# Logits of the last chunk from its hidden values and (w_out w_gate), with part of its rows made later

## The chip, the cores and the metric

The kernel runs on one core of one Trainium2 chip. The metric is the device time of one execution in microseconds (us), less is better. TensorE (PE) multiplies, VectorE (DVE) and ScalarE (ACT) work element by element, GpSimd (POOL) does too and issues indirect transfers, SyncE (SP) issues the plain ones. Line numbers (L1206) are those of the kernel before.

## The reference

```python
x = attention(q, k, v, proj)                 # (1536, 512)
h = np.maximum(x @ w_in, 0.0)                # (1536, 2048)
x = h * h @ w_out                            # (1536, 512): the rows y
logits = x @ w_gate                          # (1536, 8)
# Greedy routing by descending logit: each token goes to one expert,
# at most 192 tokens to an expert, ties in index order.
out[mask] = np.maximum(x[mask] @ w1[e], 0.0) @ w2[e]
```

## The kernel before, in words

All of it is one program in three stages: attention, the first layer (h and y), and the eight experts with the routing. The change lies in the first layer and at its join with the experts.

**First layer.** The 1536 tokens are done in four chunks of 384 (`HALF`). A chunk goes over 16 tiles f of 128 hidden columns; g = 16 c + f counts them through. For each tile TensorE does `hidden` (twelve matmuls of 384 columns, L925: two-part products of a weight split in high and low parts) into bank PB[g % 2], and `rows` (nine matmuls of 512 columns, L1206: three token tiles times three part products) which add up in PB[2] to PB[4] over all 16 tiles. The order on TensorE is hidden(g+1), then rows(g). Between the two stand, for each tile:

- ScalarE (`tile`, L929): relu out of the bank (L931) and its square, rounded to the high part h_hi (L933); then the high part of the w_in columns of tile g+2 (L942) and of the w_out rows of tile g+1 (L945). `split_parts` holds these parts, two buffers each.
- VectorE (`hidden`, L1120): the exact square h from the relu (L1122), and h_lo = h - h_hi (L1125), which `rows` waits for (semaphore hls). Both inputs of both instructions are in SBUF.
- GpSimd (`both_low`, L993): the low part of the w_in columns (L949) and of the w_out rows (L953), each one tensor_tensor of 128x512.

In the first tiles of the next chunk ScalarE copies the finished rows out (L1079), TensorE turns them (`turn`, L1220), VectorE copies the columns (L1130), TensorE makes their logits with w_gate (`logits`, L1228), VectorE copies those into L (L1134), and SP stores the rows in HBM (`y_rows`, L986). After the last chunk the same is done with nothing beside it: copies L1114 and L1116, twelve transposes L1281, twelve fp32 matmuls L1289, and the store L989. VectorE also fills the routing's tables, between the fourth and the fifth tile of the last chunk (L1169 to L1180); GpSimd its masks at the end (L1036 to L1049).

**Experts.** A new block starts, at which the engines join. VectorE chooses each token's best expert (L1516 to L1528). The first route goes in 13 steps (`STEPS`): for five digit levels TensorE counts with twelve small matmuls (L1698) what VectorE compared (L1540), VectorE answers (L1548), one more small matmul (L1700); then the places (L1666) and the token list (L1673). TensorE waits for VectorE in most steps; after steps 10 and 11 `keep_warm(5)` has five matmuls that nothing reads (L1778). GpSimd gathers the tokens' rows from `y_rows` (L1406) once all rows are stored and the list is there; SP loads the expert's weights into the places of w_in and w_out. Then TensorE runs expert after expert (L1755, L1769), with the later routes laid into it.

## Time and profile before

| | before |
| --- | --- |
| median of 3 runs | 800.35 us (800.28 to 800.99) |
| the profiled execution | 801.0 us |
| its span in the trace | 799.2 us |
| TensorE, VectorE, ScalarE, GpSimd busy | 97%, 46%, 47%, 50% |
| mean granted TensorE clock | 0.979 of full |

The span is the time from the first to the last instruction of the profiled execution; 1.8 us of the execution's own time lie around it. A line of a timeline has the start, the duration, the engine, the kernel line, what is written and read, and in brackets how long the engine had been idle and what ended that. "x2" is a merged pair. The attention takes the first third, the first layer runs from about 265 to 547 us, the experts from 552 us on.

### The profile page before, as it was taken

The page shows a single profiled execution, that of the slowest core. Times are in us where ns is not written, and L with a number is a line of the kernel's source. Part 1 is how long each engine was busy: PE and PEld are TensorE (multiplying, and loading weights), DVE is VectorE, ACT ScalarE, POOL GpSimd, SP SyncE. Part 2 cuts the span into 40 slices and gives each one's busy share as a digit, 9 for nine tenths or more (in the row PEclk, how much of TensorE's full clock was granted, in tenths as well). Part 3 has the DMA queues.
Part 4 walks back from the last instruction along what each step waited for, and adds up shares of the span by engine and source line. Part 5 has one row for each costly group of instructions (what it writes and reads, how often), then busy time and mean ns, then how long its engine had stood idle before and what let it go on. Part 6 is the DMA issues. An engine that isn't in the chain of part 4 may idle for free. (4 is left out here: it accounts for less than half of the span.)

```text
span 799.2 us, 13812 instructions
## 1 busy us (share of the span) xinstructions
PE 771.8 (97%) x4616; PEld 701.0 (88%) x4618; DVE 368.9 (46%) x852; ACT 378.5 (47%) x663; POOL 399.9 (50%) x326
## 2 busy tenths in 40 slices
PE   7999999999999999999999999997699999999996
PEld 5889889888988888999999999996399999999996
DVE  7576666666754454242242225224654554454000
ACT  2677767777677555545554554552021222122221
POOL 5577777777685787555555665562100110011101
PEclk9999999999999999999999999997599999999999
DMA  7576677665544000010010001001264743654731
GB/s 158 133 174 149 149 159 169 135 152 149 126 111 142 0 1 0 2 40 0 0 39 0 0 0 41 0 0 40 73 224 166 249 147 132 226 187 165 264 136 40
DMA packets 44220, 81.44 MB, mean 102 GB/s; under 512 B 17192, under 2 KB 17192, under 8 KB 43664
## 3 DMA queue, kind: packets, MB, share of 16 engines
q1 hardware_dynamic: 41968, 74.58, 33.0%
q0 software_dynamic: 2048, 6.29, 2.3%
q8 instruction: 25, 0.41, 0.2%
q14 instruction: 19, 0.16, 0.1%
q10 hardware_dynamic: 160, 0.00, 0.0%
HBM read 54.55 MB, written 6.29 MB: 76 GB/s over the span
## 5 line engine op out<-in xcount | busy, mean ns | idle before, releaser
L311 POOL TENSOR_TENSOR pt_lo<-pt,pt_hi 128x768 fp32r<-128x768 f32 x64 | 117.8, 1846 | 52.9 <-ACT pt_hi L444 45.7
L925 PE MATMUL banks<-xt_hi,split_parts 128*128 128x384 f32 (+1 forms) x512 | 141.3, 337 | 0.5 <-POOL split_parts L949 0.5
L949 POOL TENSOR_TENSOR split_parts<-w_in_sb,split_parts 128x512 fp32r<-128x512 f32 x64 | 85.0, 1328 | 85.5 <-ACT split_parts L942 84.2
L1122 DVE TENSOR_TENSOR h<-relu 128x384 f32<-128x384 f32 x64 | 42.9, 671 | 177.3 <-ACT relu L931 177.2
L1206 PE MATMUL banks<-split_parts,h_hi 128*128 128x512 f32 x384 | 120.6, 395 | 0.2
L437 ACT ACTIVATE pt<-banks 128x768 f32<-128x768 f32 x96 | 78.1, 813 | 65.8 <-PE banks L700 56.1
L558 DVE TENSOR_REDUCE mx<-banks 128x1 f32<-128x768 f32 x96 | 90.4, 956 | 25.0 <-PE banks L727 21.0
L925 PEld LDWEIGHTS banks<-xt_hi,split_parts 128*128 128x128 f32 x512 | 93.5, 188 | 3.5 <-issue 0.9
L1755 PE MATMUL banks<-x_cols,w_in_sb 128*128 128x192 f32 x512 | 92.6, 333 | 0.4 <-ACT x_cols L1450 0.4
L1769 PE MATMUL banks<-expert_hidden,w_out_sb 128*128 128x192 f32 x512 | 92.2, 332 | 0.0
L953 POOL TENSOR_TENSOR split_parts<-w_out_sb,split_parts 128x512 fp32r<-128x512 f32 x64 | 84.4, 1319 | 13.7 <-ACT split_parts L945 13.7
L925 PE MATMUL banks<-xt_lo,split_parts 128*128 128x384 f32 (+1 forms) x256 | 86.1, 336 | 0.0
L1755 PEld LDWEIGHTS banks<-x_cols,w_in_sb 128*128 128x128 f32 x512 | 82.4, 191 | 2.4 <-issue 0.8
L1769 PEld LDWEIGHTS banks<-expert_hidden,w_out_sb 128*128 128x128 f32 x512 | 83.1, 191 | 0.6
L1206 PEld LDWEIGHTS banks<-split_parts,h_hi 128*128 128x128 f32 x384 | 70.4, 188 | 13.3 <-DVE h_lo L1125 1.4
L1413 POOL DMA_INDIRECT out<-expert_out,rows_of_out x14 | 13.2, 946 | 135.7 <-ACT expert_out L1465 133.6
L1206 PE MATMUL banks<-split_parts,h_lo 128*128 128x512 f32 x192 | 75.8, 395 | 0.0
L931 ACT ACTIVATE relu<-banks 128x384 f32<-128x384 f32 x64 | 31.5, 492 | 86.7 <-PE banks L925 86.6
L699 PE MATMUL banks<-qa,ka 128*128 128x384 f32 x192 | 69.4, 361 | 0.8 <-ACT pt L437 0.7
L700 PE MATMUL banks<-qb,kb 128*128 128x384 f32 x192 | 64.4, 335 | 0.0
L945 ACT ACTIVATE split_parts<-w_out_sb 128x512 fp32r (+1 forms) x64 | 40.5, 632 | 41.0 <-PE banks L1206 41.0
L727 PE MATMUL banks<-kb,qb 128*128 128x384 f32 x200 | 53.0, 358 | 3.8 <-issue 1.6
(231 smaller groups left out, 1297.2 us busy)
## 6 DMA issues: line engine op xcount, KB each, us to landing
w_out_sb<-in_moe_w SPq DMA_DIRECT2D x8, 2048.0 KB, 9.0
w_in_sb<-in_moe_w SPq DMA_DIRECT2D x7, 2048.0 KB
w_in_sb<-in_moe_w_in SPq DMA_DIRECT2D x8, 512.0 KB, 6.7
w_out_sb<-in_moe_w_out SPq DMA_DIRECT2D x8, 512.0 KB, 6.1
w_out_sb<-in_k SPq DMA_DIRECT2D x16, 192.0 KB, 3.7
w_out_sb<-in_q SPq DMA_DIRECT2D x16, 192.0 KB, 4.0
v_raw<-in_v SPq DMA_DIRECT2D x16, 192.0 KB, 3.4
ka<-split_parts SPq DMA_DIRECT2D x16, 192.0 KB, 3.0
```

The source lines that it names most:

```text
L311: pool.tensor_tensor(pt_lo[x % 2][:], pt[j % 2][:], pt_hi[x % 2][:].bitcast(fp32), ALU.subtract).then_inc(los, 1)
L437: act.activation(halves(pt[j % 2]), both(ST), ACT.Exp, scale=SCALE).then_inc(ex, 1)
L558: dve.tensor_reduce(mx[:, j:j + 1], both((PREP, SM)[j % 2]), AX.XY, ALU.max).then_inc(mxs, 1)
L699: pe.matmul(ST[:, h, 0:HALF], ka[i][:, kc], qa[i][:, c], start=True, stop=False)
L700: last = pe.matmul(ST[:, h, 0:HALF], kb[i][:, kc], qb[i][:, c], start=False, stop=True)
L727: last = pe.matmul(slot[:, h % 2, 0:HALF], qb[i][:, qcol], kb[i][:, h % 2 * HALF:(h % 2 + 1) * HALF], start=True, stop=True)
L925: last = pe.matmul(PB[i][:, 0:HALF], w_[:, k, :], x_[:, xs], start=n == 0, stop=n == 3 * DT - 1)
L949: pool.tensor_tensor(wil[i], in_view(f), wih[i].bitcast(fp32), ALU.subtract).then_inc(wils, 1)
L953: pool.tensor_tensor(wol[i], out_view(f), woh[i].bitcast(fp32), ALU.subtract).then_inc(wols, 1)
L1206: last = pe.matmul(PB[2 + t][:], h_[:, tc], w_[:], start=start and n == 0, stop=stop and n == 2, skip_group_check=True)
L1755: last = pe.matmul(PB[2 + f % 2][:, 0:CAP], w1s[i][:, k, f * P:(f + 1) * P], xgt[:, k, :], start=k == 0, stop=k == DT - 1)
L1769: last = pe.matmul(PB[4 + d % 2][:, 0:CAP], w2s[i][:, f, d * P:(d + 1) * P], hs[:, f, :], start=f == 0, stop=f == F2T - 1)
```

## The change

1. A product G = w_out w_gate (2048 x 8) is made by VectorE from `w_out_sb` and a copy of w_gate's rows in all partitions (`gate_rows_sb`, a load of 2 MB by SP in chunk 0): 128 `tensor_tensor_reduce` of 128x512, each with a `drain`, three after each tile's `hidden` in chunks 0 to 2 (none in the first four tiles of chunk 0; 3, 0, 3 and 4 in those of chunks 1 and 2). G is then split into two parts (`wogs`).
2. In the last chunk TensorE adds up the logits from the squared relus' two parts times `wogs`: two matmuls of 384 columns per tile (`gate_sums`) into PB[7]. After the last tile ScalarE copies them, three small matmuls join the two parts and turn the sums, VectorE copies the logits. The last chunk's own turning, copies and logit matmuls go.
3. In the last chunk `rows` is done for tiles 0 to 8 only. For tiles 9 to 15 the h parts and w_out parts are kept (`kept`, `late_parts`, in the freed space of xt_hi and xt_lo), the latter made earlier, after tiles 2, 3, 5, 6, 8, 10 and 12. Their 63 products (`late_rows`) are made under the last tile (8), beside the logits' joining (2) and ahead of the route's steps (`FILL`).
4. The last chunk's rows are copied and stored token tile by token tile within the first route; the gather waits for these stores. The keep-warm matmuls after step 10 go, those after step 11 stay. The tables' and masks' making is spread over the last chunk's tiles. The loops of VectorE over the chunks and the last chunk's loops are written out.

```diff
+F0 = 9
+REST = FT - F0
+LATE_PARTS = {2: 9, 3: 10, 5: 11, 6: 12, 8: 13, 10: 14, 12: 15}
+PRODUCTS = 3 * CT * REST
+AHEAD = 8
+FILL = (15, 1, 6, 1, 5, 1, 5, 1, 5, 1, 4, 12, PRODUCTS)
+STORED = 16 * (CHUNKS - 1 + CT)
...
+    last_g = (CHUNKS - 1) * FT
+    def kept(f):
+        d = f - F0
+        if d >= REST - 2:
+            return split["hh"][f % 2][:], hl[f % 2][:]
+        at = DT * S + d * S if d < DT else (REST - 2) * DM
+        return xt_hi[:, at:at + HALF], xt_lo[:, at:at + HALF]
+    def late_parts(f):
+        d = f - F0
+        if d >= REST - 2:
+            return split["woh"][f % 2], split["wol"][f % 2]
+        return xt_hi[:, d * DM:(d + 1) * DM], xt_lo[:, d * DM:(d + 1) * DM]
...
+    def late_rows(pe, first, last):
+        for x in range(first, min(last, PRODUCTS)):
+            t, r = divmod(x, 3 * REST)
+            f, n = divmod(r, 3)
+            f += F0
+            if t == 0 and n == 0:
+                pe.wait_ge(hls, last_g + f + 1)
+                pe.wait_ge(late_wols, f - F0 + 1)
+            h_hi, h_lo = kept(f)
+            w_hi, w_lo = late_parts(f)
+            h_, w_ = ((h_hi, w_hi), (h_hi, w_lo), (h_lo, w_hi))[n]
+            done = pe.matmul(PB[2 + t][:], h_[:, t * P:(t + 1) * P], w_, start=False, stop=r == 3 * REST - 1, skip_group_check=True)
+            if r == 3 * REST - 1:
+                done.then_inc(row_tile, 1)
...
+            sp.wait_ge(rows_done, 4)
+            sp.dma_start(gate[:], gate_rows.unsqueeze(0).broadcast_to([P, E, DM])).then_inc(gate_in, 16)
...
-            sp.wait_ge(y_tile, CT)
-            sp.dma_start(y_rows[last:last + HALF, :].rearrange("(t p) d -> p t d", p=P), ysb[:]).then_inc(stored, 16)
...
+            for f in range(FT):
+                both_low(last_g + f, f + 2 if f + 2 < FT else None, f + 1 if f + 1 < F0 else None, f % 2)
+                if f in LATE_PARTS:
+                    x = LATE_PARTS[f]
+                    pool.wait_ge(late_wohs, x - F0 + 1)
+                    w_hi, w_lo = late_parts(x)
+                    pool.tensor_tensor(w_lo, wo[:, x * DM:(x + 1) * DM], w_hi.bitcast(fp32), ALU.subtract).then_inc(late_wols, 1)
...
+            def last_chunk():
+                for f in range(FT):
+                    g, i = last_g + f, f % 2
+                    if f < F0:
+                        act.wait_ge(rows_done, g + 1)
+                        split["tile"](act, g, i)
+                    else:
+                        act.wait_ge(hls, g - 1)
+                        split["tile"](act, g, i, kept(f)[0])
+                    if f + 2 < FT:
+                        in_high(g + 2, f + 2, i)
+                    if f == 0:
+                        chunk_rows(CHUNKS - 2)
+                    if f + 1 < F0:
+                        out_high(g + 1, f + 1, 1 - i)
+                    if f in LATE_PARTS:
+                        x = LATE_PARTS[f]
+                        if x >= FT - 2:
+                            act.wait_ge(rows_done, last_g + F0 + 2)
+                        act.activation(late_parts(x)[0], wo[:, x * DM:(x + 1) * DM], ACT.Copy).then_inc(late_wohs, 1)
...
-            act.wait_ge(stored, 16 * (CHUNKS - 1))
-            for t in range(CT):
-                act.wait_ge(row_tile, t + 1)
-                act.activation(ysb[:, t, :], PB[2 + t][:], ACT.Copy).then_inc(y_tile, 1)
-            act.wait_ge(ytp, (CHUNKS - 1) * CT + 2)
-            act.activation(yt[1][:], PB[6][:].rearrange("p (k c) -> p k c", k=DT), ACT.Copy).then_inc(y_cols, 1)
...
+            def gate_parts(n):
+                for _ in range(n):
+                    f, e = divmod(next(columns_of), E)
+                    if f == 0 and e == 0:
+                        dve.wait_ge(gate_in, 16)
+                        dve.wait_ge(split["w_early"], 16 * 9)
+                        dve.wait_ge(split["w_ready"], 16 * 8)
+                    dve.tensor_tensor_reduce(made[:], wo[:, f * DM:(f + 1) * DM], gate[:, e, :], 1.0, 0.0, ALU.mult, ALU.add,
+                                             wog[:, f, e:e + 1])
+                    dve.drain()
...
+                    if c < CHUNKS - 1:
+                        gate_parts((3, 0, 3, 4)[j])
             def rest(c):
-                with dve.Fori(2, FT // 2) as fp:
-                    hidden(c * FT + 2 * fp, 0)
-                    hidden(c * FT + 2 * fp + 1, 1)
-            chunk(0, True)
-            rest(0)
-            with dve.Fori(1, CHUNKS - 1) as c:
-                chunk(c, False)
+                for f in range(4, FT):
+                    hidden(c * FT + f, f % 2)
+                    gate_parts(3)
...
+            dve.tensor_copy(wogs[:, :, 0:E], wog[:])
+            dve.drain()
+            dve.tensor_tensor(wogs[:, :, E:2 * E], wog[:], wogs[:, :, 0:E].bitcast(fp32), ALU.subtract).then_inc(gated, 1)
...
+            def gate_sums(f):
+                g = last_g + f
+                if f == 0:
+                    pe.wait_ge(gated, 1)
+                    pe.wait_ge(logits_out, CHUNKS - 2)
+                pe.wait_ge(hls, g + 1)
+                for n, h_ in enumerate((hh[f % 2][:], hl[f % 2][:]) if f < F0 else kept(f)):
+                    last = pe.matmul(PB[7][0:2 * E, P:P + HALF], wogs[:, f, :], h_, start=f == 0 and n == 0, stop=f == FT - 1 and n == 1,
+                                     skip_group_check=True)
+                if f == FT - 1:
+                    last.then_inc(gate_done, 1)
...
+            def last_chunk(x0):
+                c = CHUNKS - 1
+                for f in range(FT):
+                    g, i = last_g + f, f % 2
+                    if f + 1 < FT:
+                        hidden(g + 1, x0, 1 - i)
+                    else:
+                        late_rows(pe, 0, AHEAD)
+                    if f == 0:
+                        pe.wait_ge(ysbs, c)
+                    if f == 1:
+                        logits(c - 1, 0)
+                        turn(c - 1, 2)
+                    elif f == 2:
+                        logits(c - 1, 1)
+                        logits(c - 1, 2)
+                    gate_sums(f)
+                    if f < F0:
+                        rows(g, i, f == 0, False)
+                    if f == 0:
+                        turn(c - 1, 0)
+                        turn(c - 1, 1)
...
-            pe.wait_ge(logits_out, CHUNKS - 1)
-            for t in range(CT):
-                pe.wait_ge(y_tile, t + 1)
-                for k in range(DT):
-                    last = pe.transpose((PB[5], PB[6], PB[0])[t][:, k * P:(k + 1) * P], ysb[:, t, k * P:(k + 1) * P], ident[:])
-                last.then_inc(ytp, 1)
-            for t in range(CT):
-                if t == 1:
-                    pe.wait_ge(y_cols, 1)
-                else:
-                    pe.wait_ge(yts, (CHUNKS - 1) * CT + (1 if t == 0 else 2))
-                for k in range(DT):
-                    last = pe.matmul(PB[7][:, t * E:(t + 1) * E], yt[t][:, k, :], wg[:, k, :], start=k == 0, stop=k == DT - 1)
-            last.then_inc(logit, 1)
...
+            for t in range(CT):
+                sp.wait_ge(y_tile, t + 1)
+                at = (CHUNKS - 1) * HALF + t * P
+                sp.dma_start(y_rows[at:at + P, :], last_rows[t]).then_inc(stored, 16)
...
+            act.wait_ge(gate_done, 1)
+            act.activation(gate_sums, PB[7][0:2 * E, P:P + HALF], ACT.Copy).then_inc(sums_out, 1)
+            for t in range(CT):
+                act.wait_ge(row_tile, t + 1)
+                act.activation(last_rows[t], PB[2 + t][:], ACT.Copy).then_inc(y_tile, 1)
...
-                    if l == 1 and not past(s, 1):
-                        dve.wait_ge(stored, 16 * CHUNKS)
...
+            dve.wait_ge(logit, 1)
+            dve.tensor_copy(L[:, NT - CT:NT, :].rearrange("p t e -> p (t e)"), PB[5][:, 0:CT * E])
+            dve.drain()
...
+            late_rows(pe, AHEAD, AHEAD + 2)
+            pe.wait_ge(sums_out, 1)
+            for t in range(CT):
+                last = pe.matmul(PB[5][:, t * E:(t + 1) * E], gate_sums[:, t * P:(t + 1) * P], both_parts, start=True, stop=True)
+            last.then_inc(logit, 1)
+            at = AHEAD + 2
-            for k in range(STEPS):
+            for k, fill in enumerate(FILL):
+                late_rows(pe, at, at + fill)
+                at += fill
                 routing(0, k)
-                if 2 * NL <= k < STEPS - 1:
+                if k >= 2 * NL and at >= PRODUCTS and k < STEPS - 1:
                     keep_warm(5)
...
+    arrays["in_gate_rows"] = _np.ascontiguousarray(inputs["moe2_w_gate"].T)
```

The kernel also gets w_gate transposed, as one more input.

## Rows read from the trace of the kernel before

**Rows 1.** The page's head: span, busy time by engine, granted TensorE clock in 40 slices.

```profile
span 799.2 us, 13812 instructions
...
PE 771.8 (97%) x4616; PEld 701.0 (88%) x4618; DVE 368.9 (46%) x852; ACT 378.5 (47%) x663; POOL 399.9 (50%) x326
...
PEclk9999999999999999999999999997599999999999
```

**Rows 2.** Timeline of one steady tile: start us, us, engine, operation [idle before].

```profile
455.28 0.49 ACT L931 ACTIVATE relu<-banks 128x384 f32<-128x384 f32 x1 [1.41 <-PE banks L925]
...
455.81 0.56 DVE L1122 TENSOR_TENSOR h<-relu 128x384 f32<-128x384 f32 x1 [2.97 <-ACT relu L931]
...
456.44 0.56 DVE L1125 TENSOR_TENSOR h_lo<-h,h_hi 128x384 fp32r<-128x384 f32 x1
...
457.04 1.30 POOL L949 TENSOR_TENSOR split_parts<-w_in_sb,split_parts 128x512 fp32r<-128x512 f32 x1 [1.63 <-ACT split_parts L942]
457.11 0.34 PE L925 MATMUL banks<-xt_hi,split_parts 128*128 x1
...
458.30 1.28 POOL L953 TENSOR_TENSOR split_parts<-w_out_sb,split_parts 128x512 fp32r<-128x512 f32 x1
...
459.02 0.34 PE L925 MATMUL banks<-xt_hi,split_parts 128*128 x1
...
459.19 0.63 PE L1206 MATMUL banks<-split_parts,h_hi 128*128 128x512 f32 x2
...
459.45 0.49 ACT L931 ACTIVATE relu<-banks 128x384 f32<-128x384 f32 x1 [1.42 <-PE banks L925]
...
459.98 0.56 DVE L1122 TENSOR_TENSOR h<-relu 128x384 f32<-128x384 f32 x1 [2.98 <-ACT relu L931]
```

**Rows 3.** Timeline of VectorE alone at the head of the second chunk.

```profile
339.46 1.42 DVE L1122 TENSOR_TENSOR h<-relu 128x384 f32<-128x384 f32 x1 [2.98 <-ACT relu L931]
340.95 1.48 DVE L1125 TENSOR_TENSOR h_lo<-h,h_hi 128x384 fp32r<-128x384 f32 x1
```

**Rows 4.** Timeline of GpSimd alone over the same stretch.

```profile
339.17 1.30 POOL L953 TENSOR_TENSOR split_parts<-w_out_sb,split_parts 128x512 fp32r<-128x512 f32 x1 [1.34 <-ACT split_parts L945]
340.69 1.32 POOL L949 TENSOR_TENSOR split_parts<-w_in_sb,split_parts 128x512 fp32r<-128x512 f32 x1 [0.23 <-ACT split_parts L942]
341.97 1.61 POOL L953 TENSOR_TENSOR split_parts<-w_out_sb,split_parts 128x512 fp32r<-128x512 f32 x1
```

**Rows 5.** Groups by line and form, VectorE: xcount | busy us, mean ns.

```profile
L1130 DVE COPY y_t<-banks 128x512 f32<-128x512 f32 x10 | 6.6, 681 | 2.9 <-PE banks L1281 2.9
...
L1589 DVE TENSOR_TENSOR members_of_expert<-members_and_ties,expert_onehot 128x192 f32<-128x192 f32 x7 | 2.5, 358 | 0.6
...
L1518 DVE TENSOR_TENSOR chosen<-logits,best 128x96 f32<-128x96 f32 x7 | 1.8, 259 | 0.5
...
L1598 DVE SCALAR_TENSOR_TENSOR logits<-open_or_filled,logits 128x96 f32<-128x96 f32 x7 | 1.8, 250 | 0.0
```

**Rows 6.** Timeline of VectorE, second and fifth tile of the last chunk.

```profile
480.81 0.93 DVE L1122 TENSOR_TENSOR h<-relu 128x384 f32<-128x384 f32 x1 [2.97 <-ACT relu L931]
...
497.24 0.56 DVE L1122 TENSOR_TENSOR h<-relu 128x384 f32<-128x384 f32 x1 [0.43 <-ACT relu L931]
```

**Rows 7.** Timeline from the last chunk's end to the first route.

```profile
546.52 1.51 PE L1281 MATMUL banks<-ident,y_rows_sb 128*128 128x128 f32 x12
...
551.24 0.18 DVE L1134 COPY logits<-banks 128x24 f32<-128x24 f32 x1 [2.48 <-PE banks L1289]
...
554.60 1.02 PE L1698 MATMUL banks<-chosen,reaches 128*128 128x8 f16 x12 [3.40 <-DVE reaches L1540]
```

**Rows 8.** Chain of waits, the same TensorE line once the experts run.

```profile
585.75 0.65 PE banks L1698 x12
```

**Rows 9.** Windows: length, busy us (xcount) PE, PEld, DVE, ACT, POOL, then granted clock, DMA share, GB/s.

```profile
578.00:579.00 1.00, 0.65 (x3) 0.10 (x1) 0.87 (x2) 0.00 (x0) 0.00 (x0) 1.00 0.63 176
```

**Rows 10.** The page's DMA issues: KB each, us to landing.

```profile
w_out_sb<-in_moe_w SPq DMA_DIRECT2D x8, 2048.0 KB, 9.0
```

More of the change, by code:

```diff
@@ L3 @@
 from contextlib import ExitStack
+from itertools import count
 B, NH, S, D = 2, 8, 768, 64
@@ L927, in hidden, with tile @@
         last.then_inc(hid, 1)
-    def tile(act, g, i):
+    def tile(act, g, i, square=None):
         act.wait_ge(hid, g + 1)
@@ L975, in first_layer @@
         ysb = sb("y_rows_sb", [P, CT, DM])
-        yt = [sb(f"y_t{i}", [P, DT, P]) for i in range(3)]
-        row_tile, y_tile, y_cols = (sem("first_" + n) for n in ("row_tile", "y_tile", "y_cols"))
+        yt = [sb(f"y_t{i}", [P, DT, P]) for i in range(2)]
+        gate = sb("gate_rows_sb", [P, E, DM])
+        made = sb("gate_products", [P, DM])
+        wog = sb("gate_of_hidden", [P, FT, E])
+        wogs = sb("gate_of_hidden_parts", [P, FT, 2 * E], f32r)
+        gate_in, gated, gate_done = (sem("first_" + n) for n in ("gate_in", "gated", "gate_done"))
         (hls, rows_done, ysbs, ytp, yts, logit, logits_out, counted, inverted, divided, head_high, head_low) = (
@@ L1124, in hidden @@
                 dve.wait_ge(hhs, g + 1)
-                dve.tensor_tensor(hl[i][:], h32[i][:], hh[i][:].bitcast(fp32), ALU.subtract).then_inc(hls, 1)
+                dve.tensor_tensor(low, h32[i][:], high.bitcast(fp32), ALU.subtract).then_inc(hls, 1)
+            columns_of = count(0)
+            def gate_parts(n):
[8 more added lines that the diff above has]
+                    dve.drain()
             def columns(c, t):
@@ L1197, in hidden, with rows @@
                 split["hidden"](pe, g, x0, i)
-            def rows(g, i, start, stop, by_tile=False):
+            def rows(g, i, start, stop):
                 pe.wait_ge(hls, g + 1)
@@ L1225, in logits, with chunk @@
                     pe.wait_ge(logits_out, c)
-                pe.wait_ge(yts, c * CT + t + 1)
+                beside = isinstance(c, int) and c == CHUNKS - 2
+                pe.wait_ge(yts, c * CT + (t + 2 if beside and t == 0 else t + 1))
+                at = PB[6] if beside else PB[7]
                 for k in range(DT):
-                    last = pe.matmul(PB[7][:, t * E:(t + 1) * E], yt[t % 2][:, k, :], wg[:, k, :], start=k == 0, stop=k == DT - 1)
+                    last = pe.matmul(at[:, t * E:(t + 1) * E], yt[t % 2][:, k, :], wg[:, k, :], start=k == 0, stop=k == DT - 1)
                 if t == CT - 1:
                     last.then_inc(logit, 1)
-            def chunk(c, x0, x_next, first, last):
+            def gate_sums(f):
[31 more added lines that the diff above has]
+                        turn(c - 1, 1)
+            def chunk(c, x0, x_next, first):
                 g0 = c * FT
@@ L1804, in _, with build @@
                 last.then_inc(last_row, 1)
-def build(nc, q, k, v, proj, w_in, w_out, w_gate, w1, w2, out):
+def build(nc, q, k, v, proj, w_in, w_out, w_gate, w1, w2, gate_rows, out):
     y_rows = nc.dram_tensor("y_rows", [TOK, DM], fp32).ap()
@@ L1847, in build @@
                 K = routing_constants(nc, shared)
-                first_layer(nc, block, sem, PB, ident, K, finish, low_done, xt_hi, xt_lo, split, wg, L, stored, y_rows, later, h32, hl)
-            experts(nc, PB, ident, K, wi, wo, L, stored, y_rows, w1, w2, out)
+                gate_sums = split["r32"][0][0:2 * E, :]
+                late = first_layer(nc, block, sem, PB, ident, K, finish, low_done, xt_hi, xt_lo, split, wg, L, stored, y_rows, later, h32, hl,
+                                   wi, wo, gate_rows, both_parts)
+            experts(nc, PB, ident, K, wi, wo, L, stored, y_rows, w1, w2, out, last_rows, both_parts, gate_sums, late)
 _INS = ("q", "k", "v", "proj", "moe_w_in", "moe_w_out", "moe2_w_gate", "moe2_w1", "moe2_w2")
```

132 lines of the change are left out of this document (69 added, 63 removed).

## The prediction

> **What bounds the kernel now.** I read the page's head first [rows 1]: TensorE is busy 97% of the span, VectorE 46%, GpSimd 50%, and the granted clock is full except in two slices, the 28th and 29th of 40. A slice is 20 us, so that dip, from 540 to 580, is the join between first layer and experts. VectorE, which gets the new work, looks half free. An average says nothing about one tile, so the timeline comes next.
>
> A steady tile [rows 2]: relus start at 455.28 and 459.45, a period of 4.17 us. TensorE fills it. The twelve hidden matmuls are (459.02 - 457.11) / 11 = 0.174 us apart, 2.08 us; the nine row products take the other 2.09, 0.232 each. VectorE does two tensor_tensors of 0.56 (L1122, L1125), from 455.81 to 457.00, and then idles 2.97 us. GpSimd's two subtracts (L949, L953) run from 457.04 to 459.58, exactly in VectorE's hole. The h_lo written at 457.00 is read at 459.19, so VectorE may be some 2 us late before TensorE notices.
>
> The reader is to see next what happens when these two engines do meet. At the head of the second chunk L1122 takes 1.42 instead of 0.56, L1125 1.48 [rows 3]. Beside them GpSimd's L953 ends at 340.47 and L949 at 342.01 [rows 4]; L1122 ends at 340.88 and L1125 at 342.43, each 0.41 to 0.42 after a GpSimd end. VectorE did nothing while the GpSimd instruction ran, then did its whole data pass. The third GpSimd instruction in turn took 1.61, 0.32 over its 1.29. So a two-input VectorE instruction and a GpSimd tensor_tensor exclude each other, whole instruction by whole instruction: VectorE loses 1.48 - 0.56 = 0.92 per GpSimd instruction met.
>
> **Part 1, 128 products of w_out and w_gate on VectorE.** Each is a 128x512 fp32 product with an accumulated sum. No such instruction is in the trace. Two-input forms cost 0.259 at 96 elements, 0.358 at 192 [rows 5] and 0.56 at 384 [rows 2], about 1.04 ns an element, so 512 give an estimate of 0.69. With the 0.07 to 0.08 between dependent VectorE instructions (L1122 to L1125 begin 0.63 apart) I take 0.78. The low end is 0.69, the high 0.93 if reading out the sum costs as much again as a small instruction's fixed part (0.259 less 96 elements, 0.16).
>
> Alone, a tile would need 1.26 (two instructions and gaps) + 3 x 0.78 = 3.60 us, and fit into 4.17. But GpSimd's two subtracts lie in just that hole, and both are met: 3.60 + 2 x 0.92 = **5.44 us a tile**, 1.27 over. Bounds: the shared resource must serve 2 x 1.25 (GpSimd, back to back), 2 x 0.42 and 3 x 0.55, together 4.99, so at least 0.82 over; if each meeting costs a full 1.25 and each product 0.93, 1.26 + 2.79 + 2.5 = 6.55, 2.4 over. I take 1.27, from the row of an actual meeting. The 2 us of slack are used once; then h_lo is late for the row products, and TensorE waits every tile.
>
> The Trainium skill, page "SBUF — State Buffer", section "Who interferes with whom", says that a VectorE instruction with two SBUF inputs contends with a GpSimd instruction that reads SBUF. It is not limited to tensor_tensor, so by it the accumulating form is caught as well and the sum stands; if it did not hold for that form, the tile would stay 4.17. The trace agrees for tensor_tensor (0.92 us a meeting) and shows nothing for the other form.
>
> Tiles: 12 with three products in each of chunks 0, 1 and 2: 36 x 1.27 = 45.7. The first four tiles of chunks 1 and 2 carry ten products (3, 0, 3, 4): VectorE needs 8 x 0.63 + 10 x 0.78 + three column copies of 0.68 [rows 5] + 0.2 + 8 x 0.92 = 22.4, against one tile of 4.17 and 497.24 - 480.81 = 16.43 for three [rows 6], 20.6. That is 1.8 twice, 3.6. The two preparing instructions before chunk 3 are 0.4. Less the slack of 2.0: **+47.7 us**.
>
> **Part 2, the last chunk.** 63 row products leave it, 8 of them are made under tile 15: 55 x 0.232 = -12.8. The 32 gate sums stream 384 columns like a hidden matmul: 32 x 0.174 = +5.6. Tiles 9 to 15 now have 2.08 + 0.35 = 2.43 us of TensorE each, while relu, square and split follow each other on ScalarE and GpSimd (relu at 455.28 to L949's end at 458.34 is 3.06 us, and the weights are wanted two tiles on), and two of them carry an extra 1.28 us GpSimd subtract, which VectorE also meets. The bounds are 0 and 7 x 1.2; I take +3.0, two tiles of about 1.5. Tiles 0 to 8 last 4.52 and hold the extra subtracts and the constants behind the slack of h_lo: nothing, and 1.3 each for the five if that slack is gone.
>
> **Part 3, the tail.** From the first transposition at 546.52 to the logits' copy at 551.24 is 4.72 us [rows 7]. In its place: a ScalarE copy like L931's 0.49, three fp32 matmuls of two passes (six at 1.51 / 12 = 0.126 each, 0.76), hand-offs of 0.1: -3.4. The engines' join between the blocks stays.
>
> **Part 4, the first route.** L1698's twelve matmuls take 1.02 us at 554.60 [rows 7], and 0.65 later at full clock [rows 8]. With 53 long products put into the gaps TensorE should not slow down, worth 0.37 a level at most; but fills of 5 or 6 products (1.16, 1.39 us) are about as long as the gaps they fill, so VectorE's next compare is answered a little late. I take -1.0, between -3 and +2.
>
> **Costed at nothing.** The new load of 2 MB into gate_rows_sb: such loads land in 9.0 us [rows 10], it is issued in tile 2 and wanted after tile 4; if late, VectorE stalls by some 2 us. On SP the y_rows stores now stand ahead of the first expert weights; the last is ready as route step 11 starts, so the weights' DMA may move by 1 us, under the list and the gather; if they were wanted at once that 1 us would show. GpSimd's gather waits for the same store, under the token list. The dropped keep-warm matmuls and transposes are covered by products.
>
> **Sum.** +47.7 - 12.8 + 5.6 + 3.0 - 3.4 - 1.0 = +39.1. The profiled execution took 801.0 (span 799.2), 0.65 above the median of the runs: 840.1 by the profile, 839.5 as a median.
>
> **The rivals.**
>
> *Faster side: the accumulating form does not exclude GpSimd.* Then 3.60 us fit into 4.17, part 1 costs nothing and the rest gives 800.35 - 8.6 = 791.8. It decides at the tile: below 0.97 us per product, contention included, nothing reaches TensorE. For: VectorE's 2.97 us hole, and no row for this form. Against: it reads two SBUF operands as L1122 does. Chance 0.14.
>
> *The meetings are mostly missed.* VectorE settles so that some GpSimd subtracts run in its waits for relu or square. But a saturated VectorE has no waits. 800 to 814, chance 0.04.
>
> *The product runs at half rate.* 512 more elements' worth, 0.53 us each: 128 x 0.53 = 68 us more, some 907. Against it, a scalar_tensor_tensor with two fp32 inputs costs 0.250 at 96 elements, no more than tensor_tensor [rows 5]; the sum's read-out is not in it. Chance 0.04. The Trainium skill, "Vector Engine (DVE) Microarchitecture Reference", section "Points that are easy to get wrong", says that this form with two non-bf16 SBUF sources halves throughput, for want of a port for the accumulator; by it this is the case to expect. The row without a read-out does not show it.
>
> *The clock falls* because TensorE idles 1.27 of 5.44 us. At 1.2 GHz a tile is 8.3 us: over 940. Against it: between 578 and 579 TensorE was busy 0.65 and held 2.4 GHz [rows 9]. Chance 0.02.
>
> **How the numbers follow.** The forecast has 0.76. Its own range, 814 to 874: 36 tiles at 0.82 over with the smaller bounds of the rest, or at 2.1 over with the larger (2.4 needs every high end at once, and is left out). Down to 806 it also holds most of the missed meetings; that makes 0.8 in all, and the range stops there; a range that took in the faster case would begin at 790. About 0.2% (1.6 us) is what a measurement can tell from no change. Faster: 0.15 (the faster rival and a little of the missed meetings); within: 0.02; slower: 0.83.
>
> **What would show it.** In chunks 0 to 2 relus 5.4 us apart instead of 4.17; TensorE at L1206 waiting for VectorE's h_lo; the product near 0.7 us alone and near 1.6 beside L949 or L953; those lengthened to 1.6 or more. The last chunk, from its first relu to the logits' copy, shorter by about 7.6 us; clock full through the first route; the experts unchanged. Wrong if relus stay 4.17 us apart with products between them: then the exclusion does not reach this form.

## The result, and the profile after

The changed kernel takes 843.45 us in the median of four runs (840.78 to 845.77), against 800.47 for the kernel before on the same chip: a ratio of 1.053 (95% interval 1.0505 to 1.0553). The forecast was 839.5. The profiled execution took 841.2 us, its span 839.5, which is 40.3 more than before (799.2). The four runs lie in two pairs, 840.8 and 841.2 (mean granted clock 0.991 and 0.990), and 845.7 and 845.8 (0.987 and 0.982): the profile shows one of the first pair, and where the second lost its 4.7 us no trace shows.

The page of the changed kernel: span, busy time, granted clock, and three of its costliest groups (xcount | busy us, mean ns | idle before, and what ended it).

```profile
span 839.5 us, 13936 instructions
...
PE 782.8 (93%) x4613; PEld 699.5 (83%) x4615; DVE 538.8 (64%) x1109; ACT 377.1 (45%) x663; POOL 423.6 (50%) x326
...
PEclk9999999999999989999999999999999999999999
...
L1292 PE MATMUL banks<-split_parts,h_hi 128*128 128x512 f32 x342 | 111.6, 408 | 33.4 <-DVE h_lo L1193 33.4
L1205 DVE CUSTOM_DVE_ANT_0 gate_products<-w_out_sb,gate_rows_sb 128x512 f32<-128x512 f32 x128 | 134.7, 1052 | 9.8
L960 POOL TENSOR_TENSOR split_parts<-w_in_sb,split_parts 128x512 fp32r<-128x512 f32 x64 | 96.6, 1509 | 69.8 <-ACT split_parts L953 69.1
```

Against [rows 1], TensorE fell from 97% to 93% of a longer span, and VectorE rose from 46% to 64%, far from full by this average. Yet TensorE waited 33.4 us for VectorE's h_lo. The product lasts 1.05 us in the mean; L1205 stands in the trace as CUSTOM_DVE_ANT_0. GpSimd's same subtract went from 1.33 to 1.51. The dip of the clock at the join [rows 1] is gone and a small one has come earlier.

Line numbers of after: the row products are L1292 (L1206), h L1190 (L1122), h_lo L1193 (L1125), GpSimd's subtracts L960 and L964 (L949, L953), relu L942 (L931), the route's counts L1812 (L1698). The timeline of one steady tile, to be laid beside [rows 2]:

```profile
403.64 0.49 ACT L942 ACTIVATE relu<-banks 128x384 f32<-128x384 f32 x1 [1.42 <-PE banks L936]
...
404.30 0.68 DVE L1205 CUSTOM_DVE_ANT_0 gate_products<-w_out_sb,gate_rows_sb 128x512 f32<-128x512 f32 x1
...
404.91 0.08 DVE L1205 DVE_READ_ACCUMULATOR2_ANT gate_of_hidden<- 128x1 f32 x1
...
405.39 1.56 POOL L960 TENSOR_TENSOR split_parts<-w_in_sb,split_parts 128x512 fp32r<-128x512 f32 x1 [1.43 <-ACT split_parts L953]
...
405.92 1.59 DVE L1205 CUSTOM_DVE_ANT_0 gate_products<-w_out_sb,gate_rows_sb 128x512 f32<-128x512 f32 x1
...
407.58 0.56 DVE L1190 TENSOR_TENSOR h<-relu 128x384 f32<-128x384 f32 x1
407.70 1.57 POOL L964 TENSOR_TENSOR split_parts<-w_out_sb,split_parts 128x512 fp32r<-128x512 f32 x1 [0.75 <-ACT split_parts L956]
...
408.21 1.48 DVE L1193 TENSOR_TENSOR h_lo<-h,h_hi 128x384 fp32r<-128x384 f32 x1
...
408.93 0.49 ACT L942 ACTIVATE relu<-banks 128x384 f32<-128x384 f32 x1 [1.41 <-PE banks L936]
...
409.74 0.50 PE L1292 MATMUL banks<-split_parts,h_hi 128*128 128x512 f32 x1 [0.91 <-DVE h_lo L1193]
```

Relus are 5.29 us apart instead of 4.17. VectorE has no gap. Two of its five instructions in a tile meet a GpSimd subtract: the third product (1.59 instead of 0.69) and h_lo (1.48 instead of 0.56). They end 0.56 and 0.42 us behind GpSimd's end; in [rows 3, 4] it was 0.41 and 0.42. The two subtracts are also longer, by about 0.28. A product alone is 0.68 or 0.69, its read-out 0.08, and products start 0.80 to 0.82 apart.

Where the 40.3 us lie, by relu starts and the start of the logits' copy (L1134 before, L1762 after); the differences are from times with three decimals:

| stage | before | after | difference | forecast |
| --- | --- | --- | --- | --- |
| chunk 0 | 70.8 | 85.7 | +14.9 | |
| chunk 1 | 70.7 | 86.0 | +15.4 | |
| chunk 2 | 70.7 | 86.0 | +15.4 | +47.7 for the three |
| last chunk to the logits' copy | 75.1 | 69.7 | -5.4 | -7.6 |
| logits' copy to the end | 248.0 | 248.1 | +0.1 | -1.0 |

In the last chunk the first four relus are followed by steps of 5.47, 6.36, 5.79 and 6.20 us (4.17, 5.05, 5.45 and 5.93 before); from tile 4 to tile 10 they are 4.5 us apart, then 2.44, 3.06, 3.42, 2.42 and 3.29. In the route the late row products (L1004) stand on the chain between the counts (columns: start us, us, what):

```profile
596.08 0.11 PE banks L1814
596.19 1.50 PE banks L1004 x6
597.68 0.73 PE banks L1812 x12
```

and the chain of before in its second level, which follows the counts of [rows 7]:

```profile
555.88 0.20 PE banks L1700
...
557.28 1.02 PE banks L1698 x12
```

The twelve count matmuls take 0.73 on the chain, 1.02 before. But from the end of the small matmul to the next counts it is 1.49 us, taken up by six products, where before VectorE's answer was there after 1.20. The counts and the small matmul (0.11 for 0.20) together give back 0.38 us a level, which is what was hoped for from the clock (0.37; it is full from 594 to 600 us here, and was at its lower level from 554 to 560 before), and the fills took it.

### The profile page after: what moved, and what is told of

It reads as the page before. It is cut to its first block and busy times, and to the rows that moved or that the text cites. A ratio compares the mean times of both kernels' runs of the same rounds, so it can differ in the third digit from the quotient of the medians.

```text
span 839.5 us, 13936 instructions
## 1 busy us (share of the span) xinstructions
PE 782.8 (93%) x4613; PEld 699.5 (83%) x4615; DVE 538.8 (64%) x1109; ACT 377.1 (45%) x663; POOL 423.6 (50%) x326
## 3 DMA queue, kind: packets, MB, share of 16 engines
q0 software_dynamic: 2048, 6.29, 2.2%
## 5 line engine op out<-in xcount | busy, mean ns | idle before, releaser
L1292 PE MATMUL banks<-split_parts,h_hi 128*128 128x512 f32 x342 | 111.6, 408 | 33.4 <-DVE h_lo L1193 33.4
L1205 DVE CUSTOM_DVE_ANT_0 gate_products<-w_out_sb,gate_rows_sb 128x512 f32<-128x512 f32 x128 | 134.7, 1052 | 9.8
L960 POOL TENSOR_TENSOR split_parts<-w_in_sb,split_parts 128x512 fp32r<-128x512 f32 x64 | 96.6, 1509 | 69.8 <-ACT split_parts L953 69.1
L964 POOL TENSOR_TENSOR split_parts<-w_out_sb,split_parts 128x512 fp32r<-128x512 f32 x57 | 85.9, 1507 | 45.0 <-ACT split_parts L956 44.9
L1292 PEld LDWEIGHTS banks<-split_parts,h_hi 128*128 128x128 f32 x342 | 61.8, 190 | 54.9 <-DVE h_lo L1193 44.2
L1190 DVE TENSOR_TENSOR h<-relu 128x384 f32<-128x384 f32 x64 | 57.1, 892 | 40.6 <-ACT relu L942 37.4
L956 ACT ACTIVATE split_parts<-w_out_sb 128x512 fp32r (+1 forms) x57 | 36.1, 633 | 81.8 <-PE banks L1292 81.8
L942 ACT ACTIVATE relu<-banks 128x384 f32<-128x384 f32 x64 | 31.4, 491 | 87.6 <-PE banks L936 87.6
L1292 PE MATMUL banks<-split_parts,h_lo 128*128 128x512 f32 x171 | 67.7, 396 | 0.0
L1193 DVE TENSOR_TENSOR h_lo<-h,h_hi 128x384 fp32r<-128x384 f32 x59 | 61.9, 1049 | 4.8 <-issue 0.4
```

What stands on the lines that cost most here:

```text
L960: pool.tensor_tensor(wil[i], in_view(f), wih[i].bitcast(fp32), ALU.subtract).then_inc(wils, 1)
L964: pool.tensor_tensor(wol[i], out_view(f), woh[i].bitcast(fp32), ALU.subtract).then_inc(wols, 1)
L1193: dve.tensor_tensor(low, h32[i][:], high.bitcast(fp32), ALU.subtract).then_inc(hls, 1)
L1205: dve.tensor_tensor_reduce(made[:], wo[:, f * DM:(f + 1) * DM], gate[:, e, :], 1.0, 0.0, ALU.mult, ALU.add, wog[:, f, e:e + 1])
L1292: last = pe.matmul(PB[2 + t][:], h_[:, tc], w_[:], start=start and n == 0, stop=stop and n == 2, skip_group_check=True)
```

## The experiments

My theory: the product and GpSimd's subtract exclude each other on their access to SBUF. Rivals: VectorE is simply too full with three more instructions a tile; the clock; the other parts of the change. All ratios are against the kernel before.

**1. The same work with one SBUF input.**

```diff
-dve.tensor_tensor_reduce(made[:], wo[:, f * DM:(f + 1) * DM], gate[:, e, :], 1.0, 0.0, ALU.mult, ALU.add,
-                         wog[:, f, e:e + 1])
+dve.tensor_reduce(wog[:, f, e:e + 1], wo[:, f * DM:(f + 1) * DM], AX.X, ALU.add)
```

> Each of the 128 products of w_out and a row of w_gate is replaced by a 128x512 tensor_reduce of the w_out slice alone: as many VectorE instructions, about as long when alone (0.7 us), but with one SBUF input. The logits of the last chunk are therefore made from sums of w_out's rows. Theory, exclusion (two SBUF inputs and GpSimd's tensor_tensor take turns): the meetings of these instructions with L960 and L964 vanish, steady relus 4.17 us apart, total 791 to 797. Rival, VectorE's plain load (its 64% share, the drains, the longer queue): steady period stays near 5.29, total 838 to 845. Rival, the accumulator's read-out is what costs: also gone here, so a fast result alone does not exclude it; the durations in the trace of the products (0.69 alone, 1.58 beside GpSimd) speak against it.

797.32 us (794.66 to 799.02), ratio 0.996 (0.9944 to 0.9971): 0.3 above the expected range, 41 below its rival's. Its timeline of VectorE and GpSimd in a steady tile:

```profile
391.58 2.20 DVE L1205 TENSOR_REDUCE gate_of_hidden<-w_out_sb 128x1 f32<-128x512 f32 x3
391.70 1.30 POOL L960 TENSOR_TENSOR split_parts<-w_in_sb,split_parts 128x512 fp32r<-128x512 f32 x1 [1.64 <-ACT split_parts L953]
392.96 1.29 POOL L964 TENSOR_TENSOR split_parts<-w_out_sb,split_parts 128x512 fp32r<-128x512 f32 x1
```

The three reductions take 0.68 each in the mean, as long as a product alone, lie beside GpSimd's two subtracts but for the first 0.12 us, and neither side is longer. The steady tiles are as before but for two of chunk 0 (5.07, 5.40). So the number and length of VectorE's instructions are not the cause. The reduction lacks three things that the product has: the second SBUF input, the 128x512 written to SBUF, and the read-out. Experiment 4, which keeps the last two, tells them apart. The Trainium skill, "SBUF — State Buffer", section "Who interferes with whom", names the first of the three: with at most one SBUF input (outside some modes) VectorE does not contend with GpSimd, with two it does. The trace agrees: 0.68 with one, 1.59 with two.

**2. None, one or two products a tile.** In place of (3, 0, 3, 4) and 3; the G that is not made is filled from other values, so the last chunk's logits are not those of the reference.

```diff
-                        gate_parts((3, 0, 3, 4)[j])
+                        gate_parts((N, 0, N, N)[j])
...
-                    gate_parts(3)
+                    gate_parts(N)
```

> No product is made; the table of products is filled once by a copy out of gate_rows_sb, so the last chunk's logits are not the reference's. Everything else of the change stays. It prices parts 2 to 4 alone. Theory: chunks 1 and 2 as in the kernel before (70.7 us each), the last chunk and tail about 8 us shorter than before (5.4 as measured with the queue's backlog, some 3 us more without), total 791 to 794. If the rest of the change were itself harmful: 800 or more.

> One product a tile (42 in all, table otherwise filled by a copy, logits of the last chunk not the reference's). Theory: one product and two meetings, 1.26 + 0.81 + 2 x 0.92 = 3.9, fit into 4.17; only the tiles after GpSimd's long instructions in chunk 0 may slip: 794 to 798 against 794.3 without products and 816.2 with two. Rival, proportional (22 us for the 84 products of two a tile, 0.26 each): 805.

> Two products a tile instead of three (84 in all, the rest of the table filled by a copy; logits of the last chunk not the reference's). Theory, exclusion: the steady period is 5.29 less one product alone (0.81) = 4.48, 0.31 over TensorE's 4.17; 36 tiles make 11 us over the version without products, 803 to 808 in all. Rival, plain load without meetings: 1.26 + 2 x 0.81 = 2.9 fits into 4.17, same time as without products. Rival, proportional (each product costs the same 46 / 128 = 0.36 us): 792 + 84 x 0.36 = 822.

None: 794.28 us (794.05 to 794.77), ratio 0.992 (0.991 to 0.9939). One: 797.02, 0.995 (0.9936 to 0.9969). Two: 816.2 (814.44 to 818.56), 1.021 (1.0193 to 1.0226). The first is 0.3 above its range, the second inside, the third 8 us above. Of the steps expected, the steady tiles did as worked out: the twelve of chunk 1 take 53.98 us, 4.50 each (expected 4.48). They take it as a pattern of 4.17, 5.4 and 5.6, not evenly, so only the mean is as worked out. The rest was chunk 0, which grew by 8.2 us instead of 4, 4.8 of them in the four steps from tile 6 on, where GpSimd has two more long instructions (L1060 and L1066, 1.96 and 2.09 us in the trace of after), and the heads of the other chunks (0.7, 1.5 and 2.3). So the price is a threshold, as expected, and not proportional: the first product a tile costs 2.7 us in all (1.0 in the first layer of the profiled execution), the second 19, the third 27. With one product the timeline shows who waits:

```profile
392.83 0.68 DVE L1205 CUSTOM_DVE_ANT_0 gate_products<-w_out_sb,gate_rows_sb 128x512 f32<-128x512 f32 x1
392.95 1.72 POOL L960 TENSOR_TENSOR split_parts<-w_in_sb,split_parts 128x512 fp32r<-128x512 f32 x1 [1.22 <-ACT split_parts L953]
```

Here VectorE came first by 0.12 us; its product keeps its 0.68, and the subtract takes 1.72 instead of 1.30. The exclusion works both ways: who comes second waits.

**3. The products alone, in the kernel before.** 128 products at the same places, both inputs from w_out_sb, nothing reads them.

```diff
+                    dve.tensor_tensor_reduce(made[:], wo[:, f * DM:(f + 1) * DM], wo[:, e * DM:(e + 1) * DM], 1.0, 0.0, ALU.mult, ALU.add,
+                                             wog[:, f, e:e + 1])
+                    dve.drain()
```

> The kernel before with only the 128 VectorE products added, in the same places (w_out slice times another w_out slice, both in SBUF; nothing reads the sums; no 2 MB load). Theory: the whole loss sits in part 1, steady period 5.3, total 800.5 + 45 to 47 = 845 to 848, and the rest of the change is a gain of 6 us. Rival, the loss needs the rest of the change (the new load, the late rows): total under 830.

852.38 us (849.24 to 853.18), ratio 1.063 (1.0603 to 1.066), some 4 us above what was expected. TensorE waits 31.7 us for h_lo and falls to the lower clock four times, for 3.4 us each, in the first layer (once, for 6.8, in after). The products alone thus cost 52 us, 47 of them in the three chunks, and the rest of the change gives back 9 of it (852.4 to 843.5); by per_tile_0 it gives 6.2. The loss lies in part 1 alone.

**4. The same products with one operand in PSUM.** ScalarE copies a slice of w_out into a free bank, once for eight products. In `psum` 108 of the 128 read the bank.

```diff
+                        w_f = PB[5 + b % 2][:]
...
-                    dve.tensor_tensor_reduce(made[:], wo[:, f * DM:(f + 1) * DM], gate[:, e, :], ...
+                    dve.tensor_tensor_reduce(made[:], w_f, gate[:, e, :], ...
...
+                    act.activation(PB[5 + b % 2][:], wo[:, f * DM:(f + 1) * DM], ACT.Copy).then_inc(copied, 1)
```

> Full computation. 108 of the 128 products (those in tiles 4 to 15) read w_out's 128x512 slice from a PSUM bank (5 or 6, idle there) into which ScalarE copies it once for its 8 products (16 copies of about 0.6 us, in ScalarE's idle time); the 20 products at the heads of chunks 1 and 2 stay as they are. The instruction, its length and its accumulator read-out are the same; only one of its two SBUF inputs is gone. Theory, exclusion: steady period 4.17, heads at most 1.8 us over each, total 792 to 799, faster than the kernel before. Rivals, plain load or read-out: steady period near 5.3, total about 840.

805.18 us (801.6 to 810.27), ratio 1.006 (1.0034 to 1.0078). The groups of its products, from SBUF and from a bank:

```profile
L1235 DVE CUSTOM_DVE_ANT_0 gate_products<-banks,gate_rows_sb 128x512 f32<-128x512 f32 x108 | 74.3, 688 | 11.8 <-issue 11.2 <-ACT banks L1144 0.6
L1235 DVE CUSTOM_DVE_ANT_0 gate_products<-w_out_sb,gate_rows_sb 128x512 f32<-128x512 f32 x20 | 20.8, 1039 | 1.6
```

108 products beside GpSimd with a mean of 688 ns, what one takes alone, in the very kernel where the 20 from SBUF take 1039. Output and read-out are the same in both groups, so the second input from SBUF is what GpSimd's subtracts meet. The mechanism is shown without changing the arithmetic, and of the 49.2 us that the products cost in the changed kernel (843.45 less per_tile_0's 794.28) 38.3 are gone. The expected 792 to 799 was missed. The remaining cost sits where VectorE is late. A few tiles of 5.0 to 5.4, in which h or h_lo themselves meet GpSimd, make 3.8 us each in chunks 0 and 2. The head of chunk 1, with ten of the 20 SBUF products and 3.4 us of lower clock, costs 4.0; that of chunk 2, with the other ten, costs nothing; and that of the last chunk, behind three late products, 3.2.

**5. Where the remainder sits.** `psum_spread` has 125 products from banks in tiles 3 to 15, 11 of them in the last chunk, 3 from SBUF, and waits once for each copied slice. `psum_spread_fill` is the same with fewer row products ahead of the route's steps.

```diff
-FILL = (15, 1, 6, 1, 5, 1, 5, 1, 5, 1, 4, 12, PRODUCTS)
+FILL = (14, 1, 5, 1, 4, 1, 4, 1, 4, 1, 4, 13, PRODUCTS)
```

> Full computation. As psum, but waits on the copy once per bank filling instead of per product (0.16 us each saved), products only in tiles 3 to 15 (3 each), 11 of them in the last chunk's tiles 3, 4, 7 and 8, and 3 from SBUF in the first tile of chunk 1. Theory: psum's 805 was 794.3 + the 20 SBUF products at the chunk heads (about 5) + tiles in which a late VectorE met GpSimd after all (eight tiles of 5.3 to 5.4 instead of 4.17); with both gone 795 to 799, faster than the kernel before. Rival, PSUM operands or ScalarE's copies themselves cost: 803 or more again.

> psum_spread with one late row product fewer ahead of each compare step of the first route (14, 1, 5, 1, 4, 1, 4, 1, 4, 1, 4, 13 instead of 15, 1, 6, 1, 5, 1, 5, 1, 5, 1, 4, 8 effective). Theory: in the changed kernel TensorE's fills are the chain through the five levels; with each 0.23 shorter the route is up to 1.2 us shorter, 0.8 to 1.2 under psum_spread. Rival: VectorE's compare is ready no earlier, or the last tile's store comes late: same time or up to 1 us more.

804.89 us (802.98 to 806.0), ratio 1.005 (1.0032 to 1.0063), not the gain expected; and 803.1 (801.4 to 805.14), 1.003 (1.0018 to 1.0047). The fills' -1.8 in the medians is more than the 0.8 to 1.2 expected, but the route itself, from one `best` to the next, shrank only from 21.81 to 21.27. The rest is not explained by the fills: of the 3.1 us between the two profiled executions, 1.6 lie at the second chunk's head (one step of 8.78 and 7.21 us), ahead of anything that the edit touches, where psum_spread was at the lower clock for 3.4 us and psum_spread_fill was not. Tile by tile, psum_spread loses against per_tile_0 at chunk 0's tiles 8 to 13 (3.7 us), at the second chunk's head (3.6, with the three SBUF products and that fall), in the last chunk from tile 9 to 10 (1.6), and 2.8 us between the first x_cols and the end, where the clock was low for 10.2 us (psum_spread_fill: 2.4 us, 13.7).

**6. The clock behind the route.**

```diff
-                    keep_warm(5)
+                    keep_warm(11)
...
-            for k, fill in enumerate((6, 1, 4)):
+            for k, fill in enumerate((8, 1, 4)):
```

> psum_spread_fill with more matmuls that nothing reads: eleven in place of five after step 11 of the first route, eight in place of six ahead of the second route's first step. In psum_spread_fill TensorE stood idle for 1.49 us behind those five (570.3 to 571.75) and 0.47 us later on, and its granted clock was at its lower level from 573.5 to 587.2; from the first x_cols to the end took 220.5 us, where the kernels without such a stretch (before, after, per_tile_0) took 218.1 to 218.2. My theory: the idle time brought the clock down and the low clock costs those 2.4 us. It gives 800.7 us (799.5 to 802.0), clock full from the token list to the first expert, x_cols to end 218.2. Rival: the clock falls whatever TensorE is given there, or the added matmuls stand in the route's way: 803 or more.

804.2 us (800.63 to 805.88), ratio 1.004 (1.0021 to 1.0052): no gain in the median. The windows of the profiled execution show where the clock fell (length, PE, PEld, DVE, ACT, POOL, granted clock, DMA share, GB/s):

```profile
572.00:574.00 2.00, 1.80 (x14) 0.84 (x13) 1.45 (x6) 0.00 (x0) 0.00 (x0) 1.00 0.66 153
574.00:576.00 2.00, 2.00 (x16) 1.00 (x15) 1.71 (x10) 0.17 (x1) 0.35 (x1) 1.00 0.79 283
576.00:578.00 2.00, 1.31 (x15) 0.81 (x14) 0.98 (x2) 0.00 (x0) 1.69 (x2) 1.00 0.80 282
578.00:580.00 2.00, 1.27 (x9) 0.54 (x9) 1.36 (x3) 0.00 (x0) 0.00 (x1) 0.90 0.44 139
580.00:582.00 2.00, 2.00 (x22) 1.99 (x21) 0.17 (x1) 0.00 (x0) 0.00 (x0) 0.50 0.17 7
```

The fall that psum_spread_fill had at 573.2 did not come there; it came at 579.6, behind two stretches of 2 us in which TensorE was busy 1.31 and 1.27. Two waits of 0.67 and 0.73 us for VectorE were left. Of the twelve runs, 800.63 us goes with a mean granted clock of 0.996 and the five above 804.7 with 0.988 or 0.989, so the clock makes at least part of this kernel's spread. That the filled gap moved the fall to the next gap is my reading of one trace each, and not shown: the route is the same in after, per_tile_0, one_input and per_tile_1, with gaps of 1.2 and 1.5 us at its end in all four, and the clock fell there for 17.1 us in one_input and 13.7 in per_tile_1, for 3.4 in per_tile_0, and in after for 3.4 only in the next route. The same gaps were followed by a long fall in one execution and by a short one or none in another.

**7. All 128 products from banks.** `rearranged` has warm's keep-warm matmuls, no product at the second chunk's first tile, 14 in the last chunk, the slice for them copied before ScalarE's wait, and the level tables moved.

```diff
+TABLE_AT = {5: 0, 6: 1, 10: 2, 12: 3, 13: 4}
-MADE_AT = [{j: 3 for j in range(4, 16)}, {0: 3, **{j: 3 for j in range(3, 16)}}, {j: 3 for j in range(3, 16)}, {3: 3, 4: 2, 7: 3, 8: 3}]
+MADE_AT = [{j: 3 for j in range(4, 16)}, {j: 3 for j in range(3, 16)}, {j: 3 for j in range(3, 16)}, {3: 3, 4: 3, 7: 3, 8: 3, 9: 2}]
```

> warm, and the products laid out so that VectorE is never behind when it meets GpSimd: none at the second chunk's first tile (three read SBUF there), 14 instead of 11 in the last chunk (tiles 3, 4, 7, 8, 9), their first w_out slice copied into its bank ahead of the wait that held it for 3.5 us, and the level tables made in tiles 5, 6, 10, 12 and 13. All 128 products then read a PSUM bank. My theory (a product from a bank is free wherever VectorE has time): the second chunk's head goes from 5.39, 7.21 back to 5.1, 5.5 us (-2.0), the last chunk's step from tile 9 to 10 from 6.05 to 4.5 (-1.5), 3.5 us below warm: some 797 us (795.5 to 799), faster than the kernel before (800.5). Rival: VectorE is full in the last chunk whatever the order, and what is taken from the second chunk's head comes back there: the same as warm, 800 to 801.

800.42 us (798.52 to 802.92), ratio 0.999 (0.9975 to 1.0006): 3.8 below warm as expected, but warm itself had missed. The second chunk's head is 5.41, 5.46 as expected, and the step from tile 9 to 10 is 4.49. But the last chunk's second step became 7.06 (5.38 in warm), and that from tile 11 to 12 became 3.82 (3.08). The timeline of VectorE and GpSimd there:

```profile
478.66 3.13 DVE L1304 CAST gate_of_hidden_parts<-gate_of_hidden 128x112 fp32r<-128x112 f32 x1
478.72 3.01 POOL L1099 IOTA iota_slots<- 128x2304 f16 x1
...
481.87 0.28 DVE L1306 TENSOR_TENSOR gate_of_hidden_parts<-gate_of_hidden,gate_of_hidden_parts 128x112 fp32r<-128x112 f32 x1
```

**8. The cast and the tables moved.** `rearranged_2`:

```diff
-TABLE_AT = {5: 0, 6: 1, 10: 2, 12: 3, 13: 4}
+TABLE_AT = {5: (0,), 6: (1,), 14: (2, 3), 15: (4,)}
...
+                    if (c, f) == (CHUNKS - 2, FT - 1):
+                        gate_parts(1)
+                        split_gate(slice(0, FT - 2))
+                        gate_parts(MADE_AT[c][f] - 1)
...
-            for k, fill in enumerate((8, 1, 4)):
+            for k, fill in enumerate((11, 1, 7)):
```

> rearranged with three things moved. Its trace shows that the cast of the G parts took 3.13 us where it met GpSimd's iota of 3.01 (0.22 in warm, where it ended before), which made the last chunk's first step 7.06 instead of 5.38 us; it now stands before the second of the last three products of the third chunk, 1.6 us earlier. The last three level tables took 1.44 us each beside GpSimd's subtracts (0.36 in warm's tiles 8 and 9) and held the kept parts back (tile 10 to 11: 3.83 for 3.08); they go to tiles 14 and 15, where GpSimd has ended. And the matmuls that nothing reads ahead of the second route's steps become 11, 1, 7 (8, 1, 4): in rearranged TensorE still waited 0.67 and 0.72 us there and the clock fell behind it. My theory: -1.7 for the cast, -0.8 for the tables, and up to -1.5 in the mean for the clock: 797.0 us (796 to 798.5), faster than the kernel before (800.6). Rival: what is taken from one place comes back at the next meeting, and the clock falls anyway: 799.5 to 801.

797.2 us (796.15 to 799.34, five runs), ratio 0.9956 (0.9942 to 0.997) to 800.55: faster than both kernels, by 3.4 and 46 us, with the same arithmetic as the change. It also keeps the shorter fills of experiment 5 and the eleven matmuls of experiment 6. Its products:

```profile
L1256 DVE CUSTOM_DVE_ANT_0 gate_products<-banks,gate_rows_sb 128x512 f32<-128x512 f32 x128 | 88.1, 688 | 11.8 <-issue 2.8 <-ACT banks L1162 0.7
```

The step of 7.06 is 5.38 again, which is the -1.7 expected. The tables' -0.8 came only in part: tile 11 to 12 (the 10 to 11 of the expectation) still takes 3.79, the next 3.40 instead of 3.78. The rival has its share there: where rearranged had a table beside a subtract (1.43 us) ahead of an h of 1.64 and an h_lo of 0.56, here h and h_lo stand earlier and both meet one (1.64 and 1.49). The gain by the clock isn't separated from these: in the profiled execution, the slowest of the five, the clock still fell, for 6.8 us within the first route (23.3 us instead of 21.3), and stayed full from the second route's first step on; of the five runs the fastest, 796.15, has a mean clock of 0.999, this one 0.992. The room that is left is some 3 us, to per_tile_0's 794.3.

## Why the prediction was right, by its own steps

**The steady tile.** Right in mechanism, and 0.15 too long: 5.44 forecast, 5.29 measured. The exclusion reaches the new form (experiments 1, 3 and 4), two meetings a tile, each at the forecast price. The product was put at 0.78 with its gap (0.81 measured) and two meetings at 0.92 each (0.90 and 0.92). From start to start the five instructions take 0.80, 0.82, 1.66, 0.63 and 1.40, together 5.31. The gap that was put too long is the one behind h_lo: unmet, a product starts 0.48 after it (395.74 less 395.27 with the reduction in one_input is 0.47), not 0.63.

**The three chunks.** 45.6 us for the three chunks, 47.7 forecast. In chunk 1 the twelve later steps cost 12.1 us (15.2 forecast: the first two were still at 4.17, as the tiles of the head, longer for other reasons, give VectorE its slack back in each chunk, and I had used it once), the head 3.2 (1.8 forecast). Chunk 0 cost about as much (14.9) in another way, which is luck: four of its twelve steps are still 4.17, seven are 5.26 to 6.17, and one is 10.48 us. Its windows (columns as above):

```profile
297.93:302.00 4.07, 0.70 (x2) 0.60 (x3) 3.81 (x7) 1.53 (x3) 1.78 (x2) 0.77 0.00 0
302.00:304.00 2.00, 2.00 (x6) 1.55 (x5) 1.81 (x5) 0.00 (x0) 0.00 (x0) 0.50 0.00 0
304.00:306.00 2.00, 2.00 (x7) 1.68 (x6) 1.81 (x5) 0.45 (x1) 0.00 (x0) 0.50 0.00 0
```

TensorE waited 3.47 us for h_lo behind three meetings in a row, was busy 0.70 of 4.07 us, and was then at its lower level, 1.2 GHz, for 6.8 us. The rival that the clock falls was given 0.02 for all tiles, and a steady tile with 0.9 us of waiting did keep 2.4 GHz; but in one place it was real, and in before_products in four.

**The last chunk and the tail.** -5.4 instead of -7.6. The first four steps cost +3.2; in per_tile_0, with the gate sums and without products, they cost +0.9. VectorE comes into the chunk late from the products of the chunk before, and "nothing" for that was wrong by 2.3 us. The stalls of tiles 10 to 15 are 2.5 (3.0 forecast). From the last relu to the logits' copy, 8.69 became 4.25.

**The route.** +0.1 instead of -1.0: within its range of -3 to +2, and for the reason named there (fills as long as the gaps). psum_spread_fill's shorter fills took 0.5 us off the route.

**Costed at nothing.** No wait for the new 2 MB load or for the stores came up among the larger waits.

**The sum.** By the profiled executions 840.1 was forecast and 841.2 measured, but the three chunks were put 2.1 us too high, the last chunk 2.2 and the route 1.1 too low: that these errors cancel is luck. The median is 2.2 us above the profiled execution by the two runs with the lower mean clock, for which the sum has no term.

**The half-rate rival** falls: 0.69 us alone for 512 elements plus 0.08 for the read-out. The Trainium skill, "Vector Engine (DVE) Microarchitecture Reference", section "Points that are easy to get wrong", says for the shape `S2S2D2_STT` (by the page's own table that of scalar_tensor_tensor) that two non-bf16 SBUF sources halve the throughput. Carried over to this instruction, as the prediction did, it would have had about twice the 0.69; here the measurement decides against that. Whether it holds for a scalar_tensor_tensor that adds up its sum, no run here shows.

**The faster rival** (the form doesn't exclude) falls by the 1.59 beside 0.69; its time, 791.8, was near what the rest of the change gives without products (794.3).

## What to carry to other kernels

A half idle VectorE isn't free for two-input work from SBUF when GpSimd uses the same hole; what counts is whether both fit one after the other in a tile. Where the operand is used several times, put it in a PSUM bank, or give the instruction one SBUF input: here the bank alone was worth 38 of the 49 us that the work had cost, and with experiments 5 to 8 on top it was 46. And lay the work so that the engine isn't late at its next fixed meeting, since one late instruction pays 0.9 us at each subtract that it then meets, and stays late.

## What was not expected of the hardware

- A cast of 128x112 on VectorE, with one SBUF input and 0.22 us alone, took 3.13 us beside GpSimd's iota of 3.01, which reads nothing. An h (two inputs) beside the same iota was not longer, as the timeline of psum_spread_fill shows:

```profile
481.14 3.01 POOL L1098 IOTA iota_slots<- 128x2304 f16 x1
...
481.68 0.56 DVE L1233 TENSOR_TENSOR h<-relu 128x384 f32<-128x384 f32 x1
```

- The last three level tables (one input, 16-bit types, 128x768) took 0.35 to 0.36 us alone and 1.44 beside a subtract, while the fp32 reduction of the first experiment was not longer beside one. So there are two kinds of meetings. The Trainium skill has both in the section named above: copy, cast and tensor_scalar can enter modes in which they contend with GpSimd, while two SBUF inputs contend only with a GpSimd instruction that reads SBUF. The four durations here agree; I had read it for two inputs alone, and it cost rearranged a part of its gain.
- The lower clock has a price of its own: 10 to 17 us of it around the first expert, 6.5 to 8.3 of them behind the first x_cols, go with a stretch from there to the end of 220.5 to 221.0 us instead of 218.2. One_input and per_tile_1 (221.0 and 220.5) have the route and the experts of after and per_tile_0 (218.2), and the same gaps at the route's end, so these 2.4 to 2.8 us are not the idle time. Why the clock falls long in one execution and not in another stays open.
